# Second MoE stage: the first product's K tiles 0 and 1 by seven block products instead of eight

## The reference

```python
# 1. attention, per batch and head, over 768 time steps
state = alpha[t][:, None] * state + outer(k[t], v[t]);  y[t] = q[t] @ state
# 2. first MoE stage, w_in 384x2048, w_out 2048x384
h = x @ w_in;  x = (h * cos(h)) @ w_out
# 3. second MoE stage, w1, w2, w3 384x768, w_out 768x384
h = max(max(x @ w1, x @ w2), x @ w3);  out = h @ w_out
```

## Time and profile before

| | |
|---|---|
| median of 3 runs | 893.09 us |
| the profiled execution | 895.14 us |
| its span | 893.4 us |
| mean granted TensorE clock | 0.994 of full speed |

### The profile page before, as it was taken

One profiled execution on the slowest core, in us unless ns is written; L12 is line 12 of the kernel. 1 busy time (PEld: TensorE's weight loads), 2 busy tenths in 40 slices (PEclk: granted clock), 3 DMA queues, 4 the chain that ended last, 5 costly groups with the idle time before them and its releaser, 6 DMA issues.

```text
span 893.4 us, 12884 instructions
## 1 busy us (share of the span) xinstructions
PE 851.8 (95%) x4444; PEld 723.4 (81%) x4444; DVE 531.4 (59%) x1120; ACT 359.0 (40%) x706; POOL 216.5 (24%) x242
## 2 busy tenths in 40 slices
PE   3688899999999999999999999999999999999998
PEld 3678798888888888888888878878888888888887
DVE  8698898777778777777775466642232322333222
ACT  3675656544444444444544456521221211211211
POOL 6564243333333333333233213200000000000000
PEclk9899999999999999999999999999999999999999
DMA  9542113201320132012203003110020000100000
GB/s 244 143 110 46 48 41 74 74 14 42 73 64 14 40 72 71 14 41 67 76 14 120 1 35 89 54 72 36 0 72 1 36 36 35 35 35 0 0 36 35
DMA packets 13771, 47.14 MB, mean 53 GB/s; under 512 B 1968, under 2 KB 2480, under 8 KB 13712
## 3 DMA queue, kind: packets, MB, share of 16 engines
q1 hardware_dynamic: 12992, 42.47, 17.3%
q0 software_dynamic: 720, 3.93, 1.1%
HBM read 36.96 MB, written 9.44 MB: 52 GB/s over the span
## 4 chain that ended last, share of the span: by engine, by line
PE 48%; DVE 1%; ACT 1%; issue 0%; POOL 0%; DVEq 0%; ACTq 0%
PE h_ps L1009 6%; PE h_ps L1011 6%; PE h_ps L1010 6%; PE score L1011 4%; PE score L1010 4%; PE score L1009 4%; PE acc_pair L1009 1%; PE acc_pair L1011 1%; PE acc_pair L1010 1%; PE acc_pair L1116 1%; PE acc_pair L1118 1%; PE acc_pair L1117 1%; PE acc_last L1010 1%; PE acc_last L1009 1%; PE acc_last L1011 1%; PE y_ps L1118 1%
## 5 line engine op out<-in xcount | busy, mean ns | idle before, releaser
L1009 PE MATMUL h_ps<-x_hi,w_hi 128*128 128x512 f32 (+1 forms) x498 | 193.7, 389 | 5.1 <-DVE gated L793 2.6
L1011 PE MATMUL h_ps<-x_lo,w_hi 128*128 128x512 f32 (+1 forms) x498 | 186.1, 374 | 0.0
L1010 PE MATMUL h_ps<-x_hi,w_lo 128*128 128x512 f32 (+1 forms) x498 | 185.8, 373 | 0.0
L353 POOL TENSOR_TENSOR turns<-turns,whole 128x512 f32<-128x512 f32 x75 | 96.1, 1282 | 268.1 <-DVE whole L807 268.1
L499 ACT ACTIVATE cosine<-turns 128x512 f32<-128x512 f32 (+1 forms) x112 | 63.6, 568 | 144.0 <-POOL turns L353 115.5
L793 DVE TENSOR_TENSOR gated<-cosine,h_ps 128x512 f32<-128x512 f32 (+1 forms) x112 | 68.1, 608 | 76.1 <-ACT cosine L499 75.5
L1009 PEld LDWEIGHTS h_ps<-x_hi,w_hi 128*128 128x128 f32 x498 | 94.4, 190 | 21.3 <-DVE gated L793 3.3
L1011 PEld LDWEIGHTS h_ps<-x_lo,w_hi 128*128 128x128 f32 x498 | 93.9, 189 | 18.0
L1010 PEld LDWEIGHTS h_ps<-x_hi,w_lo 128*128 128x128 f32 x498 | 94.4, 190 | 14.2
L1009 PE MATMUL acc_pair<-g_hi,w_hi 128*128 128x512 f32 (+1 forms) x224 | 83.5, 373 | 10.2 <-POOL g_lo L360 9.0
L674 DVE RECIPROCAL inv_decay<-decay 112x128 f32<-112x128 f32 x96 | 90.2, 943 | 0.1
(11 more groups left out here) (136 smaller groups left out, 1608.5 us busy)
## 6 DMA issues: line engine op xcount, KB each, us to landing
raw<-qka SPq DMA_DIRECT2D x46, 288.0 KB, 4.8
v_pad<-val SPq DMA_DIRECT2D x24, 288.0 KB, 3.2
block_out<-x SPq DMA_DIRECT2D x6, 768.0 KB, 3.4
x_in<-block_out SPq DMA_DIRECT2D x6, 768.0 KB, 4.3
raw<-wb SPq DMA_DIRECT2D x12, 384.0 KB, 3.1
out<-raw POOLq DMA_DIRECT2D x5, 768.0 KB, 3.5
stage_own<-wa SPq DMA_DIRECT2D x6, 384.0 KB, 4.9
x<-wa SPq DMA_DIRECT2D x6, 384.0 KB, 4.7
```

Of the source, the lines that this page charges most:

```text
L353: nc.gpsimd.tensor_tensor(frac[:], turns[:], whole[:], ALU.subtract).then_inc(S["frac_done"], 1)
L1009: mm(ps, w_hi[:, w_at], xh, start=first, stop=False)
L1010: mm(ps, w_lo[:, w_at], xh, start=False, stop=False)
L1011: return mm(ps, w_hi[:, w_at], xl, start=False, stop=final)
```

## The change

`h = x @ w` is made for three weight matrices. Now two tiles of hidden rows (f = 2fp, 2fp+1) and the three matrices give six 128-row tiles, taken as three pairs r of an upper and a lower tile: r = 0 is w3 of both f; r = 1 and r = 2 are (w1, w2) of one f each. Of the three K tiles of 128, the first two are made by Strassen's scheme in Winograd's form: the block matrix [A11 A12; A21 A22] (upper and lower rows, K tiles 0 and 1) times [B11 B12; B21 B22] (K tiles 0 and 1, front and back 256 tokens) in 7 block products. The third K tile stays plain (K1, K2): 4 block products. One row pair (`row_pair`) is so 11 block products of 3 matmuls with 256 columns, where two tiles of 3 K tiles took 18 matmuls with 512. There are 3 row pairs to a pair fp, 3 pairs to a token tile, 54 in all.

The sums of weight blocks (S1 to S4) are made by GpSimd in the last step of the first stage (`weight_sums`, 4 instructions of 384 columns, at i = 2, 7, 12), the sums of token blocks (T1 to T4) by GpSimd for each tile (`token_sums`, 4 of 256 columns). Weights are now 11 blocks of 384 columns for each fp, split in 18 pieces, of which 4 come in the first token tile.

Within a row pair two banks p and q (of two such pairs in turn) hold partial sums that grow: ScalarE copies the back half of q three times and that of p once (`snapshots`, 256 columns each) into `snaps[r]`, and TensorE waits for each copy before it goes on in that bank. VectorE then adds p and q to the copies, and for r = 1, 2 takes the maximum of the two rows and of the result with the row of r = 0. `accumulate2` is cut in single token blocks (`fill`), placed between the waits, and now runs one pair fp behind. `snaps[0]` lies in `state`, `snaps[1]` and `snaps[2]` in the four work tiles.

The diff, cut to its core (the rest: buffers, the host's order of the weights, the semaphores' names, the split of `x2_in` in four parts):

```diff
+HI_AT = {3: (0,), 4: (1,), 5: (2,), 6: (3,), 7: (4,), 8: (5, 6), 9: (7,), 10: (8,), 11: (9,), 12: (10,), 13: (11,),
+         14: (12,), 15: (13,)}
+LO_AT = {i + 1: k for i, k in HI_AT.items()}
+HI_LATE, LO_LATE = {1: 14, 2: 15, 3: 16, 4: 17}, {0: 13, 1: 14, 2: 15, 3: 16, 4: 17}
+FILL = ((0, 0), (0, 1), (0, 2)), ((0, 3), (1, 0), (1, 1)), ((1, 2), (1, 3))
...
+            def weight_sums(n):
+                pool.wait_ge(S["stage2_in0"], 16 * (n + 1))
+                pool.wait_ge(S["stage2_in1"], 16 * (n + 1))
+                if n:
+                    pool.wait_ge(S["blo_done"], PIECES * (n - 1) + 4)
+                else:
+                    low_ready(pool, TILES1 - 1)
...
+                mul(s1, a21, a22, ALU.add).then_inc(S["sum_done"], 1)
+                pool.wait_ge(S["sum_done"], 4 * n + 1)
+                mul(s2, s1, a11, ALU.subtract).then_inc(S["sum_done"], 1)
+                mul(s3, a11, a21, ALU.subtract).then_inc(S["sum_done"], 1)
+                pool.wait_ge(S["sum_done"], 4 * n + 3)
+                mul(s4, a12, s2, ALU.subtract).then_inc(S["sum_done"], 1)
...
+                mul(t1, b12, b11, ALU.subtract).then_inc(S["x_sum"], 1)
+                mul(t3, b22, b12, ALU.subtract).then_inc(S["x_sum"], 1)
+                pool.wait_ge(S["x_sum"], 4 * t + 1)
+                mul(t2, b22, t1, ALU.subtract).then_inc(S["x_sum"], 1)
+                pool.wait_ge(S["x_sum"], 4 * t + 3)
+                mul(t4, b21, t2, ALU.subtract).then_inc(S["x_sum"], 1)
...
+                    if not attend and i == 1:
+                        token_sums(0)
+                    if not attend and i in (2, 7, 12):
+                        weight_sums(i // 5)
...
             with pool.Fori(0, STEPS - 1) as t:
+                token_sums(t + 1)
                 pool.wait_ge(S["o_act"], 2 * t + 2)
                 pool.wait_ge(S["o_dve"], 2 * t + 2)
...
+                if isinstance(t, int) and t == fp == 0:
+                    if r == 0:
+                        act.wait_ge(S["state_done"], 2 * UNITS * STEPS)
+                    else:
+                        act.wait_ge(S["glo_done"], TILES1 * (STEPS + 1))
+                elif r == 0:
+                    act.wait_ge(S["m_max"], 4 * pair)
+                else:
+                    act.wait_ge(S["mlo_done"], 2 * pair + r - 2)
+                for k, (to, ps, at) in enumerate(((snaps[r][:, 0, front], q, back), (snaps[r][:, 0, back], q, back),
+                                                  (snaps[r][:, 1, back], p, back), (snaps[r][:, 1, front], q, back))):
+                    act.wait_ge(S["m_part"], 4 * n + k + 1)
+                    nc.scalar.activation(to, ps[:, at], ACT.Copy).then_inc(S["m_snap"], 1)
...
+                first = isinstance(t, int) and t == 0
+                for fp in range(FPAIRS):
+                    for r in range(ROWPAIRS):
+                        if not (first and fp == r == 0):
+                            snapshots(t, s, fp, r)
+                        m = TILES2 * t + 2 * fp
+                        if r == 0 and not (first and fp == 0):
+                            m_high(m - 1, 1)
+                        if r == 2:
+                            m_high(m, 0)
+                            if fp == 0 and not first:
+                                store_out(t - 1)
+                        if first and 3 * fp + r in HI_LATE:
+                            high_piece(HI_LATE[3 * fp + r])
+                        if fp == 1 and not (isinstance(t, int) and t == STEPS - 1):
+                            for part in ((0,), (1, 2), (3,))[r]:
+                                split_high(t + 1, 1 - s, part)
...
+                first = isinstance(t, int) and t == 0
+                for fp in range(FPAIRS):
+                    pair = FPAIRS * t + fp
+                    for r in range(ROWPAIRS):
+                        n = 9 * t + 3 * fp + r
+                        p, q = m_ps[(9 * s + 3 * fp + r) % 2]
+                        row_a, row_b = snaps[r][:, 0], snaps[r][:, 1]
+                        if r == 2 and fp == 0 and not first:
+                            store_out(t - 1)
+                        dve.wait_ge(S["mp_done"], n + 1)
+                        dve.wait_ge(S["m_snap"], 4 * n + 2)
+                        nc.vector.tensor_tensor(row_a, row_a, p[:], ALU.add).then_inc(S["m_added"], 1)
+                        if r == 0 and not (first and fp == 0):
+                            m_low(TILES2 * t + 2 * fp - 1, 1)
+                        if r == 2:
+                            m_low(TILES2 * t + 2 * fp, 0)
+                        dve.wait_ge(S["mq_done"], n + 1)
+                        dve.wait_ge(S["m_snap"], 4 * n + 4)
+                        nc.vector.tensor_tensor(row_b, row_b, q[:], ALU.add).then_inc(S["m_added"], 1)
+                        if r:
+                            dve.wait_ge(S["m_added"], 2 * n + 2)
+                            nc.vector.tensor_tensor(row_a, row_a, row_b, ALU.max).then_inc(S["m_max"], 1)
+                            dve.wait_ge(S["m_max"], 4 * pair + 2 * r - 1)
+                            nc.vector.tensor_tensor(row_a, row_a, snaps[0][:, r - 1], ALU.max).then_inc(S["m_max"], 1)
+                        if first and 3 * fp + r in LO_LATE:
+                            low_piece(LO_LATE[3 * fp + r])
+                        if not (isinstance(t, int) and t == STEPS - 1):
+                            if fp == 1 and r:
+                                for part in ((0,), (1, 2))[r - 1]:
+                                    split_low(t + 1, 1 - s, part)
+                            if fp == 2 and r == 0:
+                                split_low(t + 1, 1 - s, 3)
...
+                def fill(k):
+                    if k < len(FILL[r]) and not (first and fp == 0):
+                        pos, j = FILL[r][k]
+                        accumulate2(*((t, 2 * fp - 2 + pos) if fp else (t - 1, TILES2 - 2 + pos)), j)
...
+                wait(pe, "m_added", 2 * n - 2)
+                times(q[:, front], A22, t4, True, False)
+                times(q[:, front], K2, last1, False, True)
+                times(q[:, back], A11, b11, True, True).then_inc(S["m_part"], 1)
+                times(p[:, front], A12, b21, True, False)
+                times(p[:, front], K1, last1, False, True)
+                fill(0)
+                pe.wait_ge(S["m_snap"], 4 * n + 1)
+                times(q[:, back], S2, t2, False, True, True).then_inc(S["m_part"], 1)
+                times(p[:, back], S1, t1, True, True).then_inc(S["m_part"], 1)
+                fill(1)
+                pe.wait_ge(S["m_snap"], 4 * n + 2)
+                times(q[:, back], S3, t3, False, True, True).then_inc(S["m_part"], 1)
+                pe.wait_ge(S["m_snap"], 4 * n + 3)
+                times(p[:, back], S4, b22, False, False, True)
+                times(p[:, back], K1, last2, False, True, True).then_inc(S["mp_done"], 1)
+                pe.wait_ge(S["m_snap"], 4 * n + 4)
+                times(q[:, back], K2, last2, False, True, True).then_inc(S["mq_done"], 1)
+                fill(2)
```

More of the change, by code:

```diff
@@ L89, in build @@
         x_lo = sb("x_lo", [P, 2, KT, TOK], fp32r)
-        turns = sb("turns", [P, TOK])
-        whole = sb("whole", [P, TOK])
+        work = sb("work", [P, 4, TOK])
+        turns, whole, cosine, gated = (work[:, k] for k in range(4))
         frac = turns
-        cosine = sb("cosine", [P, TOK])
-        gated = sb("gated", [P, TOK])
         g_hi = sb("g_hi", [P, 2, TOK], fp32r)
@@ L581, in step @@
                         g_high(t - 1, half)
[L582 to L587, removed]
+                    if not attend:
+                        for k in HI_AT.get(i, ()):
+                            high_piece(k)
                     cosines(t, half)
-                    if not attend and i == 2:
-                        split_high(0, 0)
+                    if not attend and 3 <= i < 7:
+                        split_high(0, 0, i - 3)
                 if attend:
@@ L1064, in _, with accumulate2 @@
             accumulate1(TILES1 - 1, TILES1 - 1, first_tokens, 0, True)
-            def product2(t, s, f, w):
-                if isinstance(t, int) and t == 0 and w == 0:
-                    pe.wait_ge(S["b_xlo"], 1)
-                    pe.wait_ge(S["blo_done"], (W2COLS // W1COLS) * (f + 1))
-                i = 3 * TILES2 * s + 3 * f + w
-                back = 3 * f + w - 4
-                wait(pe, ("m_copied", "m_max2", "m_max3")[back % 3], TILES2 * t + back // 3 + 1)
-                for k in range(KT):
-                    at = f * W2COLS + (w * KT + k) * P
-                    last = split_mm(m_ps[i % 4], slice(at, at + P), (x_hi[:, s, k], x_lo[:, s, k]),
-                                    k == 0, k == KT - 1)
-                last.then_inc(S["m_done"], 1)
+            def accumulate2(t, f, j, final=False):
+                n = TILES2 * t + f
+                pe.wait_ge(S["mlo_done"], n + 1)
+                if f == 0 and j == 0:
```

(12 more changed lines are left out.)

238 lines of the change are left out of this document (152 added, 86 removed).

## The result

The changed kernel takes 937.51 us, the median of 4 runs (929.81 to 939.2), where the kernel before, run beside it on the same chip, takes 893.42. The ratio is 1.0465, 95% interval 1.0394 to 1.0535: **slower by 4.6%**. The profiled execution took 937.99 us, its span is 936.4 and its mean granted clock 0.978, where before had 0.994. The forecast of 920 us had the right sign and named the places of the waits; the time lies 5.5 us above the upper end of the range.

The account below looks back on a forecast made before the run. The prediction took TensorE's pace to bound the second stage, with nearly no slack in the first stage's last step. Its terms, -19.5 + 24.7 + 2.7 + 4 + 2.3 + 4 + 9, gave +27.2 us: 920 us, range 895 to 932.

Parts of the forecast that it names:

- Term 1: Second stage's products: 33 matmuls of 256 columns replace 18 of 512 per row pair, at 0.116 us each; -19.5 us.
- Term 2: Pair ends: TensorE waits for ScalarE's first copy into `snaps[0]`, held by the previous pair's maxima; 17 times 1.45, +24.7 us.
- Term 3: Fourth copy of each row pair: released 0.05 us later than TensorE wants the bank, 54 times; +2.7 us.
- 4, first pair: First pair of the first tile: no `fill` to cover the copies, and VectorE has extra weight pieces; +4 us.
- Term 5: Tail: the last two output products both wait behind the last row pair; +2.3 us.
- Term 6: Tiles 1 to 4, first pair's end: VectorE's maxima wait while GpSimd runs `token_sums`; 0.9 to 1.8 us, four times, +4 us.
- Term 7: First stage's last step: GpSimd's weight and token sums delay `fraction` in the chain TensorE waits for; +9 us.
- so I count nothing: Granted clock: 0.97 seen between 45 and 100 us with TensorE busy 44.6 of 55 us; loss costed at zero.
- if `m_low` were out of the way: Lower end for the waits at pair ends: 0.6 us each, +10 us, without `m_low` between VectorE's adds.
- C: Rival: copies hide through a shorter VectorE order at the pair's end, GpSimd's sums hidden too; 880 us, chance 0.15.
- E: Rival: 256-column pace is 0.118 or worse under load and VectorE starves at every train; 932 us or more, chance 0.05.

Follow-up runs that it names:

- pause7: Kernel before the change, with 7 chained extra ScalarE copies that TensorE waits for once in each token tile: 925.24 us, ratio 1.0336.
- tsmove: Changed kernel with GpSimd making the token sums of tile t+2 before it waits for the store of tile t: 925.14 us, ratio 1.0345.
- all3: Changed kernel with a second buffer for the rows of r = 0, earlier token sums, and the last step's sums on VectorE: 884.42 us, ratio 0.9868.
- halves: Kernel before the change, with each product of 512 columns made as two of 256, nothing else: 897.04 us, ratio 1.0021.
- early: Changed kernel with `m_low` ahead of both adds of r = 2 and `m_high` between ScalarE's first and second copy: 914.21 us, ratio 1.021.
- best: Changed kernel with second buffer for r = 0, earlier token sums, last step's sums on VectorE, and `m_low` and `m_high` moved ahead: 884.02 us, ratio 0.9878.
- double: Changed kernel with a second buffer for the rows of r = 0, used by every other pair fp: 895.29 us, ratio 1.0001.

## Why the prediction was wrong, by its own steps

The difference of the spans is 936.4 - 893.4 = +43.0 us. By the prediction's terms:

| Term | forecast | measured |
|---|---|---|
| 1, columns | -19.5 | 18 x (15.87 - 16.76) = -16.0, less the 1.8 of Term 3 in it: -17.8 |
| 2, end of a pair | 17 x 1.45 = +24.7 | 17 x 1.54 = +26.2 |
| 3, fourth copy | +2.7 | 54 x 0.034 = +1.8 |
| 4, first pair | +4 | +2.0 |
| 5, tail | +2.3 | 1.16 + 1.25 - 0.25 = +2.2 |
| 6, token sums | +4 | 1.99 + 3.99 + 1.99 + 4.14 - 4 x 1.54 = +6.0 |
| 7, last step | +9 | 1.18 + 1.91 + 3.74 + 2.74 = +9.6 |
| clock | 0 | +10.6 |
| sum | +27.2 | +40.6 |

Another 1.25 us lie ahead of the last step, where this execution ran from 45 to 100 us at 0.91, not 0.97; 1.1 us are not placed. Two sizes in the table are rough and work against each other: the slower interval behind each of the 17 gaps of Term 2, 0.1 us, is not in it, and the clock's 10.6 are a tenth too many in time.

**The step that failed** is the sentence on the clock: "so I count nothing". It read the 0.97 between 45 and 100 us as what a busy share of 81% costs, and concluded that a busier stage would pay nothing. But the loss goes with single gaps. In the kernel before TensorE starts at 70.20 after a gap of 2.0 us, and its next 8 us (busy time of PE, PEld, DVE, ACT and POOL, then clock and DMA) are:

```profile
70.20:78.20 8.00, 8.00 (x54) 7.71 (x55) 7.26 (x17) 3.55 (x12) 2.44 (x2) 0.79 0.01 2
```

TensorE is busy all 8 us of it. (1 - 0.79) x 8 = 1.7 us lost in 55 is the whole 0.03. (A longer gap, up to 91.9, was not followed by half clock.) The forecast itself put gaps of 1.4 to 3.7 us into the last step and the second stage. Five stretches at half clock, after the gaps that ended at 565.94, 671.53, 728.25, 783.62 and 840.34, cost 1.7 + 1.7 + 2.6 + 1.7 + 2.9 = 10.6 us. With them the forecast would have been 930.6, inside the range. pause7 shows the cost by itself, tsmove shows it going with the gaps. The 7 us that would still be missing are no one step: 2.8 are the sizes of the other terms together, 1.25 lie ahead of the last step, and the rest is not placed.

**Term 1** was 1.7 us too large. The pace of 256 columns varies by place from 0.1134 to 0.1181 us. Start to start over the two pairs of all3, 256 columns take 0.1176 on average, or 0.1166 without the fourth copy's share, where 0.116 was taken; the 384 columns of the fills take 0.176, where they take 0.1736 before. Each of the two is about 1 us in 18 pairs; 0.5 come back, as 512 columns take 0.2332 before, not 0.2327. Why the pace varies is open; halves puts 2 ns of it down to the matmul as such. **Term 2** was right in place, cause and count; its size was 6% low, and 13% with the slower interval behind the gap, part of which the 1.45 was meant to cover. Part of it stands in the timeline at 704 us: the first add starts at T+0.03, not T-0.03, and ScalarE's copy 0.13 us behind the last maximum, not 0.03. That "if `m_low` were out of the way" the boundary costs 0.6 was tested by early: 0.64 to 1.02. **Term 3 and 4** were too high by 1 and 2 us, **Term 5 and 7** right. **Term 6** had the mechanism and the four places; it priced 0.9 to 1.8 us for each, and two of the four took 2.4 and 2.6 more, the other two 0.45. It did not ask who starts first, and at 724.05 VectorE waited for three of GpSimd's instructions. The Trainium skill (SBUF — State Buffer, two separate sides) has one lock for the port pair that an instruction keeps to its end; that VectorE did not get in between three in a row is what this trace adds.

Of the rivals, C ended up as what the kernel could have been: with the waits gone (all3) it takes 884 us, where C said 880. Its condition was not met by order, only by a second buffer. E's number, 932 or more, takes in what was measured, its cause was not met: 256 columns kept 0.117 on average, and VectorE was held long at two of the four trains.

In the last step the cause is what the prediction named, as the timeline after shows at the longest gap:

```profile
559.61 1.77 DVE L995 TENSOR_TENSOR w_lo<-raw,w_hi 128x768 fp32r<-128x768 f32 x1
...
560.65 1.61 POOL L426 TENSOR_TENSOR stage_own<-raw,stage_own 128x384 f32<-128x384 f32 x1
...
562.23 1.26 POOL L400 TENSOR_TENSOR work<-work 128x512 f32<-128x512 f32 x1
...
565.94 0.53 PE L1171 MATMUL h_ps<-x_hi,w_hi 128*128 128x512 f32 x1 [3.58 <-DVE work L928]
```

GpSimd's sums push the next `fraction` to 562.23, and `hidden1` starts at 565.94, 3.74 us after TensorE could have started it; 3.7 was the forecast's upper value for one such place. The forecast named three gaps of 2 to 4 us; there are four, and only two of them (3.74 and 2.74) are that long.

## What to carry to other kernels

Before an anti-dependence is put on a queue that was full (here a copy that waits for the last reader of its target), count what lies between the reader's operand and the overwrite. If the chain is longer than the work in between, try a second buffer first: the better of the two reorderings of `m_low` gave 23 us here, the buffer 42. Price a gap of TensorE at its length while it is short, and add 1.5 to 3 us once it is of the length that is followed by half clock, about 2 us here. A helper on GpSimd beside a critical VectorE chain should be placed where that chain is idle; its price otherwise hangs on which of the two starts first.

## What the runs showed of the hardware

- **Half clock after a gap.** In the twelve kernels, in the last step and the second stage, no gap up to 1.91 us was followed by a fall of the granted clock. Of two gaps of 1.92 us, both in the tail, one was (best: 0.50 from 879.9 to 881.4 us, early: not while TensorE worked). Of six gaps of 1.98 or 1.99 us five were (0.79 over the next 8 us), and of 23 gaps from 2.3 to 4.3 us twenty (0.62 to 0.81). In the longer ones the clock was often down before the gap had ended (0.50 from 726.8 to 728.2 in the changed kernel). The same gap at the same place does not always do it: that of 2.74 at 591.36 in the changed kernel was followed by 1.00, that of 2.75 at 591.11 in tsmove by 0.80. What decides in between stays open. The Trainium skill (TensorE: Matmul & The Clock Gate, Part 1) has the two levels, 1.2 and 2.4 GHz. The 0.213 us for 256 columns after a long gap agree with the lower one; at the upper, 0.107 us by the clock alone, the trace has 0.113 to 0.118.
- **An execution's own start.** The last step began up to 6 us earlier or later in executions of kernels that are the same up to there: the gap of Term 7 that ends at 541.09 in the changed kernel ends at 535.40 in double. The first 100 us show it in the clock (0.91 and 0.97), and it may be why double's fastest run lies 4 us below its median.
- **A train on GpSimd.** One instruction of VectorE of 0.69 us took 2.51, through three instructions of GpSimd; the fourth and the second maximum then overlapped, at 1.06 us instead of 0.74 and 1.09 instead of 0.69. That was so when the train started 0.14 us ahead of it or 0.06 behind it (2.71 us); from 0.19 us behind on, the instruction kept its 0.69 us and the next one took 1.09.
